# The order of ScalarE's pooled exponentials and copies, and the first loads over one queue

## What is computed

```python
q_d, k_d, v_d = (mean over groups of 4 positions of q, k, v)
out_up = np.repeat(sm_attn(q_d, k_d, v_d), 4, axis=2)
scores = np.where(np.abs(pos[:, None] - pos[None, :]) < 4, scale * q @ k.T, -1e9)
out_local = softmax(scores) @ v
x = out_up + out_local            # to [2304 tokens, 512]
x = ((x @ w1) * (x @ w2) @ w3) @ w_out
h = x @ w_in
out = (h * sigmoid(h)) @ w_out2
```

## Time and profile before

| | us |
|---|---|
| median of 3 runs | 818.29 |
| lowest and highest | 817.83, 820.70 |
| the profiled execution's own time | 818.61 |
| its span, first to last instruction | 816.8 |
| TensorE busy in it | 793.5 (97%) |
| VectorE, ScalarE, GpSimd busy | 594.7, 348.2, 271.8 |

### The profile page before, as it was taken

How to read it: one execution, slowest core, us unless ns; L and a number is a source line. 1 busy time by engine, 2 the same in 40 slices (tenths; PEclk the granted TensorE clock), 3 DMA queues, 4 the chain that set the end, 5 groups by cost and what they waited for, 6 DMA issues and landing times.

```text
span 816.8 us, 13915 instructions
## 1 busy us (share of the span) xinstructions
PE 793.5 (97%) x5400; PEld 716.2 (88%) x5400; DVE 594.7 (73%) x949; ACT 348.2 (43%) x791; POOL 271.8 (33%) x342
## 2 busy tenths in 40 slices
PE   7799999999999999999999999999999999999997
PEld 6678777989998999989999888888889888888986
DVE  6888886677676776886769677679677769757644
ACT  5887867532352223433245233344322344433321
POOL 7887874342214223223313122113113112212100
PEclk9999999999999999999999999999999999999999
DMA  9575643011111111111103131122322112412102
GB/s 322 162 242 199 214 126 124 26 53 53 41 37 53 52 30 49 53 44 35 52 28 129 54 101 52 52 79 94 111 77 79 52 55 78 152 52 85 45 0 78
DMA packets 23041, 69.84 MB, mean 86 GB/s; under 512 B 2496, under 2 KB 2496, under 8 KB 22976
## 3 DMA queue, kind: packets, MB, share of 16 engines
q1 hardware_dynamic: 22832, 68.36, 25.6%
q10 hardware_dynamic: 144, 0.59, 0.2%
HBM read 64.23 MB, written 4.72 MB: 84 GB/s over the span
## 4 chain that ended last, share of the span: by engine, by line
PE 85%; ACT 7%; DVE 4%; issue 2%; DMA 1%; ACTq 0%; DVEq 0%
PE ps L1034 43%; PE ps L1092 25%; PE ps L1063 12%; PE ps L1117 2%; ACT prob_d L492 2%; ACT prob L503 2%; PE ps L1192 1%; ACT pt L439 1%; DVE prob L750 1%; PE ps L1178 1%; DVE low L758 1%; DMA qk<-in_qk 1%; DVE wa L708 1%; ACT w3t L439 0%; DVE totd L782 0%
## 5 line engine op out<-in xcount | busy, mean ns | idle before, releaser
L1034 PE MATMUL ps<-xb,wa 128*128 128x384 f32 x2016 | 405.0, 338 | 0.5 <-DVE mu L862 0.4
L1034 PEld LDWEIGHTS ps<-xb,wa 128*128 128x128 f32 x2016 | 355.0, 188 | 22.6 <-DVE mu L862 1.5
L374 POOL TENSOR_TENSOR rw<-rw 128x256 f32<-128x256 f32 x192 | 166.8, 889 | 451.8 <-DMA rw<-in_sets 338.4
L862 DVE TENSOR_TENSOR mu<-ps,mu 128x384 f32<-128x384 f32 x132 | 73.1, 554 | 120.8 <-PE ps L1034 120.6
L1063 PE MATMUL ps<-g,r 128*128 128x512 f32 (+1 forms) x576 | 124.9, 338 | 2.3 <-issue 2.3
L602 ACT ACTIVATE a<-a 128x384 f32<-128x384 f32 x72 | 37.9, 526 | 188.3 <-DVE a L862 188.3
L1092 PE MATMUL ps<-w2h_even,g 128*128 128x512 f32 x432 | 113.2, 394 | 0.0
L1092 PE MATMUL ps<-w2h_odd,g 128*128 128x512 f32 x432 | 112.5, 393 | 0.0
L708 DVE TENSOR_TENSOR wa<-rw,wa 128x1024 fp32r<-128x1024 f32 x96 | 106.0, 1104 | 4.3 <-ACT wa L439 4.2
L1063 PEld LDWEIGHTS ps<-g,r 128*128 128x128 f32 x576 | 97.7, 188 | 10.9 <-issue 2.9
L1092 PEld LDWEIGHTS ps<-w2h_odd,g 128*128 128x128 f32 x432 | 79.9, 188 | 11.9
(11 more groups left out here) (78 smaller groups left out, 737.7 us busy)
## 6 DMA issues: line engine op xcount, KB each, us to landing
rw<-in_sets SPq DMA_DIRECT2D x48, 512.0 KB, 3.5
w2r<-in_w_out SPq DMA_DIRECT2D x24, 512.0 KB, 3.5
qk<-in_qk SPq DMA_DIRECT2D x15, 576.0 KB, 6.5
vg<-in_vg SPq DMA_DIRECT2D x16, 336.0 KB, 4.2
vw<-in_vw SPq DMA_DIRECT2D x16, 320.0 KB, 3.1
out<-osb SPq DMA_DIRECT2D x18, 256.0 KB, 2.8
wn<-in_w SPq DMA_DIRECT2D x16, 256.0 KB, 4.5
raw<-in_w_out SPq DMA_DIRECT2D x2, 1024.0 KB, 10.0
```

The costliest lines, as they stand in the source:

```text
L374: nc.gpsimd.tensor_tensor(blocks[:, o, :], blocks[:, a, :], blocks[:, b, :], op).then_inc(done, 1)
L862: nc.vector.tensor_tensor(o, half_bank(k, i), term, ALU.add).then_inc(sum_ready, 1)
L1034: e = nc.tensor.matmul(ps[:, (k + i) % 2, 0:TH], wa[:, k % 2, l, A_SLOT[i], a * P:(a + 1) * P], xb[:, i, r, a, :], start=(i in (0, 1, 4) a ...
```

## The change

Four things are changed. The first loads all go over SP's queue, in the order pair 0, pair 1, values of pair 0, pair 2, and ScalarE issues none. On ScalarE the pooled exponentials move in front of the w3 copy and of both copies of turned weights from step 4 on, and in steps 1 to 3 they move behind `copy_ptd`. On VectorE `totals_down` moves in front of `w3_low` from step 4 on, and in steps 2 and 3 behind the low parts of w_out. TensorE gets one more constant transpose at its start.

```diff
-            load_qk(0)
-            load_vg(0)
-            load_vw(0)
-            load_qk(2)
+            for s in range(3):
+                load_qk(s)
+                if s == 1:
+                    load_vg(0)
+                    load_vw(0)
...
-            act.dma_start(qk_at(1).rearrange("p c s -> p (c s)"), qk_in[1, :, :]).then_inc(qk_here[1], 16)
-
...
                 exps_late()
+                if s >= FOLD:
+                    exps_down()
                 for q in splits_of(s):
                     w3_high(q)
                 if s > 0:
                     copy_pt()
+                    copy_ptd()
                 if s == 0:
                     act.wait_ge(blank, 2)
-                exps_down()
-                if s > 0:
-                    copy_ptd()
+                if s < FOLD:
+                    exps_down()
...
+                if s >= FOLD:
+                    totals_down(s)
                 for q in splits_of(s):
                     w3_low(q)
-                totals_down(s)
                 for n in W_OUT.get(s - 1, ())[0::2]:
...
+                if s < FOLD:
+                    totals_down(s)
...
-            warm(8)
+            warm(9)
```

## The result

The changed kernel takes **822.39 us** (median of 16 runs, 821.0 to 824.95) against 818.6 for the kernel before beside it: 1.0043 times as long, with a 95% interval of 1.0034 to 1.0052. The forecast was 814.7 with a range of 812.5 to 817.5, so it missed by 7.7 us and in sign. The profiled execution took 823.57 us, with a span of 821.8 against 816.8. All runs compared in this document are fast ones but for a single one of e2, at 1986.9 us: it moves e2's median by 0.06 us, and as it is the profiled one, no trace of e2 is read.

A forecast was written before the change was run, and what follows sets the result against it. TensorE, mostly in the MLP stage, has 85% of the chain; attention gains pass to the end. Terms -0.8, -1.15, -1.1, -0.4 and -0.3 sum to -3.75, rounded to -3.6: 818.29 - 3.6 = 814.7 us, range 812.5 to 817.5.

The forecast's parts named there:

- a rule of turns: At the port shared by VectorE and GpSimd: whoever starts first blocks; two VectorE instructions in a row keep their turn; unsized.

The follow-up runs named there:

- e2: The kernel before with only the change's new orders of steps 1 to 3; 818.14 us, ratio 0.9989.
- e8: e7 with only the extra VectorE subtraction of steps 8 and 10 to 14 moved behind the next pair's minimum; 815.72 us, ratio 0.9957.
- e7: The changed kernel with all orders from step 4 on as before, so only new loads and orders of steps 1 to 3; 817.85 us, ratio 0.9985.
- after: The changed kernel itself, with all parts of the change, against the kernel before; 822.39 us, ratio 1.0043.
- e12: The changed kernel with the extra subtraction of steps 8 and 10 to 14 ahead of `w3_low`, right behind `totals_down`; 821.64 us, ratio 1.0036.
- e3: The kernel before with only the change's ScalarE and VectorE orders from step 4 on; 824.69 us, ratio 1.0068.
- e10: The changed kernel with the extra subtraction and, from step 4 on, `w3_low` behind the next pair's minimum; 816.59 us, ratio 0.9976.
- e9: The changed kernel with the extra subtraction of steps 8 and 10 to 14 behind the next pair's minimum; 817.80 us, ratio 0.9988.

## What to carry to other kernels

When one engine's wait is removed, look at what the instructions behind it will then run beside: here VectorE's subtractions of two SBUF tiles and GpSimd's divisions exclude each other, so being early for `totd` only meant being in time for the division. Put what the next stage waits for (here the mask and minimum, which ran beside a division undelayed) ahead of filler work that waits for it, and keep filler that covers a wait where it covers it. e8, which does the first with the extra subtraction and the second with `w3_low`, is 2.1 us below e7 and, with the loads and the first steps, 2.7 below the kernel before, where the whole change lost 3.8. And a rule of turns read off one pair of instructions is a guess until it is seen in more places.

## What was unexpected of the hardware

- **Who gets the turn between VectorE and GpSimd.** In after, e12 and e3, where a VectorE instruction had itself waited at the port, a waiting GpSimd division came each time ahead of VectorE's next subtraction (1.63 to 2.16 us where 0.66 to 1.22 is the undisturbed time). Where it had started at once, the division stood back and took 1.5 to 2.4 us instead of 1.14. But this isn't the whole rule. In step 8 of e10, `w3t` ran undisturbed (0.68) and GpSimd's shift still came ahead of `wa` (1.63):

```profile
76.34 0.68 DVE L732 TENSOR_TENSOR w3t<-wn,w3t 128x512 fp32r<-128x512 f32 x1
...
76.51 0.99 POOL L381 TENSOR_TENSOR prob<-prob,low 128x256 f32<-128x256 f32 x1 [0.80 <-DVE low L759]
76.94 1.63 DVE L709 TENSOR_TENSOR wa<-rw,wa 128x1024 fp32r<-128x1024 f32 x1
```

  And in e9's step 11, `wa`, from 100.74 on, took 2.76 us: the second division, the shift and the pooling of v ended at 101.15, 101.73 and 102.68 meanwhile. What tells these apart wasn't tried.
- **The same loads land differently.** With one queue and one order, the values of pair 0 came at 7.58 to 8.15 in seven profiles and at 9.44 in one, while pair 0 came at 4.46 to 4.67 in all.
- **The clock** fell in some executions and not in others of the same kernel, and the changed kernel's spread (821.0 to 824.95) is mostly that.
